# Attention ahead of two expert layers: attends in pairs, q asked for ahead of v, and a changed first unit

## What is computed

```python
# q, k, v: (4, 8, 576, 64), window 64
scores = q @ k.T / 8                       # per batch and head
mask = (rel >= 0) & (rel < 64)             # rel = query position - key position
attn = softmax(where(mask, scores, -1e9))
x = (attn @ v)                             # heads side by side: (2304, 512)
h = x @ w_in; x = (h * sigmoid(1.702 * h)) @ w_out       # 512 -> 2048 -> 512
# then 8 experts (512 -> 1024 -> 512), the best 2 of each token by x @ w_gate plus noise
```

## Time and profile before

| | |
|---|---|
| median of 3 runs | 992.86 us (991.76 to 993.39) |
| profiled execution | 993.39 us, its span 991.7 us |
| TensorE, matmuls | 970.2 us busy, 98% |
| VectorE | 546.6 us, 55% |
| ScalarE | 438.3 us, 44% |
| GpSimd | 484.2 us, 49% |
| attention | to about 116 us of the span |

### The profile page before, as it was taken

One profiled execution on the slowest core, in us unless ns is written; L12 is line 12 of the kernel. 1 busy time (PEld: TensorE's weight loads), 2 busy tenths in 40 slices (PEclk: granted clock), 3 DMA queues, 4 the chain that ended last, 5 costly groups with the idle time before them and its releaser, 6 DMA issues.

```text
span 991.7 us, 19802 instructions
## 1 busy us (share of the span) xinstructions
PE 970.2 (98%) x5432; PEld 844.7 (85%) x5433; DVE 546.6 (55%) x1328; ACT 438.3 (44%) x1094; POOL 484.2 (49%) x564
## 2 busy tenths in 40 slices
PE   7999999999999999999999999999999999999995
PEld 6888899999999999999998788888888888888884
DVE  4667622225225233243344887676777777767762
ACT  5899843333342342342243444443444444444431
POOL 5566678756877787787927221221221221122121
PEclk9999999999999999999999999999999999999998
DMA  7999677959999999999838525888976869494211
GB/s 176 213 220 221 122 232 257 319 166 309 341 294 328 321 316 338 318 286 291 267 114 290 175 85 160 253 268 274 258 224 207 254 181 292 135 283 140 55 57 49
DMA packets 252496, 225.25 MB, mean 227 GB/s; under 512 B 84620, under 2 KB 182412, under 8 KB 252432
## 3 DMA queue, kind: packets, MB, share of 16 engines
q1 hardware_dynamic: 214352, 185.02, 62.9%
q0 software_dynamic: 9280, 28.62, 8.1%
q10 hardware_dynamic: 28800, 10.83, 5.0%
HBM read 140.68 MB, written 85.82 MB: 228 GB/s over the span
## 4 chain that ended last, share of the span: by engine, by line
PE 94%; DVE 2%; DMA 2%; issue 1%; SPq 1%; ACT 1%; POOL 0%; POOLq 0%; ACTq 0%
PE bank L1674 22%; PE bank L1682 21%; PE bank L1571 20%; PE bank L1590 20%; PE bank L1501 3%; PE bank L1523 2%; PE bank L1485 2%; DMA q_raw<-q 2%; PE bank L1615 2%; PE bank L1509 1%; PE bank L1607 1%; DVE hT L1255 1%; PE bank L1498 1%; SPq L476 1%; DVE he L1274 0%
## 5 line engine op out<-in xcount | busy, mean ns | idle before, releaser
L1674 PE MATMUL bank<-W,xe 128*128 (+1 forms) x960 | 226.1, 391 | 0.0
L1682 PE MATMUL bank<-W,he 128*128 (+1 forms) x960 | 224.7, 389 | 1.1 <-DVE he L1274 1.1
L1674 PEld LDWEIGHTS bank<-W,xe 128*128 128x128 f32 x960 | 181.2, 189 | 37.8
L1682 PEld LDWEIGHTS bank<-W,he 128*128 128x128 f32 x960 | 179.9, 188 | 39.0 <-issue 1.9
L1590 PE MATMUL bank<-W,gs 128*128 128x512 f32 x864 | 205.8, 392 | 0.0
L1571 PE MATMUL bank<-xs,W 128*128 128x384 f32 x768 | 197.0, 337 | 0.2 <-DVE gs L1151 0.2
L1590 PEld LDWEIGHTS bank<-W,gs 128*128 128x128 f32 x864 | 161.2, 188 | 32.0
L1255 DVE STREAM_TRANSPOSE hT<-bank 32x256 f32<-32x256 f32 x320 | 144.1, 450 | 42.1 <-PE bank L1674 37.9
L1151 DVE TENSOR_TENSOR gs<-bank,gs 128x384 fp32r<-128x384 f32 x96 | 53.5, 557 | 187.2 <-ACT gs L900 187.2
L795 POOL DMA_INDIRECT out<-y_sb,yrow x40 | 41.3, 1032 | 233.5 <-DVE y_sb L1287 224.4
L958 ACT ACTIVATE hq<-bank 32x256 f32<-32x256 f32 x320 | 119.8, 374 | 67.2 <-PE bank L1674 61.4
(11 more groups left out here) (185 smaller groups left out, 1034.4 us busy)
## 6 DMA issues: line engine op xcount, KB each, us to landing
W<-split_weights SPq DMA_DIRECT2D x112, 512.0 KB
raw<-moe_w SPq DMA_DIRECT2D x128, 256.0 KB, 3.7
split_weights<-raw SPq DMA_DIRECT2D x112, 256.0 KB, 4.1
split_weights<-xT SPq DMA_DIRECT2D x99, 256.0 KB, 4.2
xg<-x_by_expert ACTq DMA_DIRECT2D x160, 64.0 KB
v_pairs<-v SPq DMA_DIRECT2D x16, 544.0 KB, 4.2
q_raw<-q SPq DMA_DIRECT2D x16, 288.0 KB, 3.7
out<-zeros SPq DMA_DIRECT2D x12, 384.0 KB, 4.5
```

What stands on the lines that cost most here:

```text
L1674: ins = nc.tensor.matmul(h2_ps[par][:, f * 512:(f + 1) * 512], xe[par][:, xl, d * P:(d + 1) * P], weights(e, wl, d * FE + f * 512), start= ...
L1682: ins = nc.tensor.matmul(ye_ps[par][:], he[par][:, hl, c * P:(c + 1) * P], weights(e, wl, W1COLS + c * DM), start=(c == 0 and wl + hl == 0 ...
```

## The change

There are three parts. TensorE makes no attend in even steps and two in each odd step, n-5 and then n-4; in the first body they begin at m = 5. SyncE asks in the bodies from i = 1 on for q of unit u+2 before v of unit u; in the first body and in the last the order stays. In unit 0 the turned k goes to banks 5 and 6 instead of 3 and 4, so its turns wait for no copy of q, and ScalarE's first instruction is a load of the table for exp.

```diff
--- before.py
+++ after.py
@@ -285,6 +285,7 @@
 
         s_ps, pt_ps, o_ps = banks[0:2], banks[5:7], [banks[2], banks[7]]
         tr_ps = [banks[3][:, 0:S // 2], banks[4][:, 0:S // 2], banks[3][:, 0:SPLIT], banks[4][:, 0:S - SPLIT]]
+        first_tr_ps = tr_ps[0:2] + [banks[5][:, 0:SPLIT], banks[6][:, 0:S - SPLIT]]
 
 
         consts_ready = sem("consts_ready")
@@ -451,11 +452,19 @@
                 yield (qT[u_par][rows_h, :, h].rearrange("c b (p e) -> c b p e", e=2)[:, :, :, e],
                        tr_ps[h][e * DH:(e + 1) * DH].rearrange("c (b p) -> c b p", b=BLOCKS))
 
-        def k_part(u_par, batch):
+        def first_unit(u):
+
+            return isinstance(u, int) and u == 0
+
+        def turned_bank(u, batch):
+
+            return (first_tr_ps if first_unit(u) else tr_ps)[batch]
+
+        def k_part(u, u_par, batch):
 
             first = tiles_of(batch)[0] * TP
             count = len(tiles_of(batch)) * TP
-            return kT[u_par][:, QB + first:QB + first + count], tr_ps[batch]
+            return kT[u_par][:, QB + first:QB + first + count], turned_bank(u, batch)
 
         @block.sync
         def _(sp):
@@ -483,9 +492,12 @@
             def unit_loads(i, par, last):
 
                 u = i * 2 + par
-                load_v(u, par)
+                if last or (isinstance(i, int) and i == 0):
+                    load_v(u, par)
                 if not last:
                     load_q(u + 2)
+                if not (last or (isinstance(i, int) and i == 0)):
+                    load_v(u, par)
                 if not (last and par):
                     load_w(i + par, 1 - par)
                 if not last:
@@ -843,7 +855,7 @@
                     for dst, src in q_parts(par, 1):
                         ins = nc.scalar.activation(dst, src, ACT.Copy, scale=SCALE)
                 else:
-                    dst, src = k_part(par, batch)
+                    dst, src = k_part(u, par, batch)
                     ins = nc.scalar.activation(dst, src, ACT.Copy)
                 ins.then_inc(turned_act, 1)
 
@@ -870,6 +882,7 @@
                     exps(n, m)
                     if not (last and m >= 3) and m % 3 < 2:
                         turned(i * 2 + m // 3 + 1, (m // 3 + 1) % 2, m % 3 + 1)
+            nc.scalar.preload_act_table(ACT.Exp)
             act.wait_ge(q_zero, 1)
             for batch in (1, 2):
                 turned(0, 0, batch)
@@ -1476,13 +1489,13 @@
                     after(pe, turned_act, u * 2)
                 if batch == 1:
                     after(pe, turned_dve, u * 2)
-                if batch == 2:
+                if batch == 2 and not first_unit(u):
                     pe.wait_ge(turned_dve, u * 2 + 1)
-                if batch == 3:
+                if batch == 3 and not first_unit(u):
                     pe.wait_ge(turned_act, u * 2 + 1)
                 src = q_raw if batch < 2 else k_raw
                 for j, t in enumerate(tiles_of(batch)):
-                    ins = nc.tensor.transpose(tr_ps[batch][:, j * TP:(j + 1) * TP], src[:, t], ident[0:TP, 0:TP])
+                    ins = nc.tensor.transpose(turned_bank(u, batch)[:, j * TP:(j + 1) * TP], src[:, t], ident[0:TP, 0:TP])
                 ins.then_inc(qk_turned, 1)
 
             def score_waits(n, u, g):
@@ -1532,7 +1545,8 @@
                         turn_p(n - 3, (m - 3) % 6)
                     score_waits(n, i * 2 + m // 3, m % 3)
                     score(m // 3, m % 3)
-                    if not (first and m < 4):
+                    if m % 2 and not (first and m < 5):
+                        attend(n - 5, i if m >= 5 else i - 1, (m - 5) % 6)
                         attend(n - 4, i if m >= 4 else i - 1, (m - 4) % 6)
                     if more and m % 3 < 2:
                         for batch in ((0, 1) if m % 3 == 0 else (2, 3)):
```

## The result

| | before | after |
|---|---|---|
| median | 992.36 us (19 runs) | 994.50 us (19 runs) |
| profiled execution | 993.39, span 991.7 | 995.07, span 993.4 |
| next stage's first matmul in the span | 116.59 us | 118.33 us |

The changed kernel is slower: ratio 1.0021, 95% interval 1.0015 to 1.0027. The forecast was 991.4; the time lies in the range of 987.0 to 996.5, but it went up where a fall was forecast. The whole difference of the two spans (1.7 us) is there when the attention ends.

The account below looks back on a forecast made before the run. TensorE was taken to set the pace, with waits for q and a slow start as further limits. Start -1.8, pairs -6.4, q -2.0, k +7.4 and +1.0, end +0.3 gave -1.5 us: 991.4 us, range 987.0 to 996.5.

Parts of the forecast that it names:

- The start, -1.8: Unit 0: early table load and separate banks for k bring the first scores 1.9 us earlier; 1.8 taken.
- Pairs, -6.4: TensorE's attends: pairing saves switches of shape, 0.29 us in each of 22 pairs, 6.4 us in all.
- The price of a switch: TensorE's attends: one costs 0.65 us with its switches of shape, a second one behind it at least 0.35.
- I cost it at nothing in the loop: ScalarE's copy of p, 0.3 us late in odd steps, costs nothing, as ScalarE has 0.6 us a unit spare.
- only at the k turn: VectorE's copy of q's turned half waits behind an attend's copy, but TensorE needs that half only at the k turn.
- Rival 3: ScalarE's late copy of p pushes exps past the next scores, 0.3 us a pair; half shows, +3, 994.5; chance 0.08.
- q, -2.0: SyncE's order in the loop: with q asked for earlier, TensorE's 2.0 us of waits for q go.
- the spacing from v to k of 2.93 us: SyncE's issues: from v to the first k 3.53 us before, 2.93 without q (about 0.6) between.
- k, +8.4: Even units' k turn waits 1.2 us for k in six places, 7.4 us; slower first rounds add about 1.
- Landing: The last k transfer in even units lands 2.5 us after its issue.
- rival 2: k binds harder: landing in 3.3 us, two units take 14.1, six waits of 2.0, some 996 us; chance 0.25.
- End, +0.3: After the loop, where the last exps lead to the last attend, ScalarE's late copy costs 0.3 us.

Follow-up runs that it names:

- e6: The changed kernel with v of units 1 to 15 brought in one transfer instead of two: 991.8 us, ratio 0.9994 to the kernel before.
- e9: The changed kernel without the pairs of attends and with v in one transfer: 991.9 us, ratio 0.9999 to the kernel before.
- e7: The kernel before with the changed start alone, and v in one transfer: 992.5 us, ratio 0.9999 to the kernel before.

## Why the prediction was wrong

- **The start, -1.8**: right, -2.2 measured by itself. In the changed kernel 1.5 us of it is there at the q turn of unit 2.
- **Pairs, -6.4**: this is the step that failed most. The price of a switch was right (0.35 for a second attend), but not that it comes through to the total: measured, the pairs are worth 0 with whole copies of q (988.2 and 988.7 us) and 3.6 with half of them. What failed is "I cost it at nothing in the loop", and the sentence that q's turned half is needed "only at the k turn": in even units that turn had moved 0.6 us nearer to the q turn. I had compared ScalarE's spare time on average, not the chain from scores over exps to the copy. Rival 3 had the engine, but put its cost on the scores, and gave it 0.08. The half copies were only tried with v left out. That the copies take the whole gain in the changed kernel too is argued from its timeline (the k turn at 65.23) and not shown by a run of its own.
- **q, -2.0**: the waits for q went as said, but the order alone costs 1.7 us. What failed is the spacing from v to k of 2.93 us, read with v ahead of q. With q just ahead of v it is 3.05 to 3.65 us in the five even units from 38 to 96 us, median 3.50 (64.84 to 68.49 is 3.65), since SyncE stands longer behind v.
- **k, +8.4**: it binds in even units as forecast, with v issued in step m=1. The waits there are 4.9 us in six, and 0.7 in two others. The forecast had more, since it let TensorE arrive earlier, with the pairs' gain. Landing was right (median 2.3 for the last, 2.5 taken), but in the chain it is the second of the 96 KB transfers that is late, 2.92 to 3.10 us after its issue. The pitch, the time of two units, is 13.67 (42.21 to 96.90, four times two units), where 13.3 was forecast and 14.1 was rival 2's. The same kernel without transfers of v has 12.80; the forecast's pieces add up to 12.0 without a wait. So the base was 0.8 too short and the wait for k some 0.4 too long.
- **End, +0.3**: 0.9 from the q turn of unit 15 to the next stage.

By the parts, -2.2 for the start and +1.7 for q first would be -0.5 us; the changed kernel is at +2.1. So, if the parts simply add, the pairs cost 2.6 us on top. Beside that stand the waits for k, 5.6 us in place of 2.4, and no gain from the pairs.

So it went rival 2's way, the slower side, but in part for a cause that I had dismissed, the copies. The range was drawn to take in the near part of rival 2, and so it held. That the time is only 3 us from the forecast is luck: two large gains stood against one large loss in the sum, neither gain was there in the total, and the loss was smaller too.

## What to carry to other kernels

A wait list tells what bound before. When work is moved closer to its input, follow the one chain from that input through every engine to it; an engine's mean spare time says nothing of that. A spacing of issues that stands behind a large transfer isn't the issuer's own: it changes with what is put ahead of it. And a change of three parts should be run in parts: here one of them, alone, was the whole gain.

## What the runs showed of the hardware

The issue that stood right behind the large transfer of v took SyncE long, whoever's it was: a median of 1.55 us (before) and 2.13 us (changed) for v's own 16 KB, up to 2.88 us there, 1.8 and 2.1 us for the 256 KB of w in e6 and e9, 1.3 us for q in e7. Most other issues took 0.3 to 0.5 us in the same timelines. The reading that a queue's fullness makes it wait fits these rows; no run measured its limit, and no run varied the fullness by itself.

In the start, scores took 1.49 us and later 0.83, at a granted clock of 1.00 in both stretches. The shorter durations came 2.7 us earlier in the start alone (11.39 against 14.13), where TensorE had fewer pauses ahead of them; why they come when they do is open.
